# Five token blocks in place of six in a sliding-window attention and two-MLP kernel

## The reference

```
q, k, v: (4, 8, 576, 64)                   # batch, heads, sequence, head size
scores = q k^T / 8 - slope_h * |i - j|,    # only for 0 <= i - j < 128
attn   = softmax(scores) v                 # -> x: 2304 tokens x 512
h = relu(x @ w_in1); x = (h * h) @ w_out1  # 512 -> 2048 -> 512
h = x @ w_in2;       out = (h * cos(h)) @ w_out2
```

## Time and profile before

| | |
|---|---|
| median of 3 runs | 913.17 us (911.78 to 913.77) |
| the profiled execution | 912.75 us, its span 910.6 us |
| TensorE matmuls | 6128, busy 894.9 us |
| VectorE, ScalarE, GpSimd busy | 518.6, 369.2, 193.7 us |
| granted TensorE clock, mean | 0.998 of full |

### The profile page before, as it was taken

One profiled execution on the slowest core, in us unless ns is written; L12 is line 12 of the kernel. 1 busy time (PEld: TensorE's weight loads), 2 busy tenths in 40 slices (PEclk: granted clock), 3 DMA queues, 4 the chain that ended last, 5 costly groups with the idle time before them and its releaser, 6 DMA issues.

```text
span 910.6 us, 17307 instructions
## 1 busy us (share of the span) xinstructions
PE 894.9 (98%) x6128; PEld 840.7 (92%) x6128; DVE 518.6 (57%) x1239; ACT 369.2 (41%) x886; POOL 193.7 (21%) x298
## 2 busy tenths in 40 slices
PE   6999899999999999999999999999999999999998
PEld 4888799999999999999999989999999899999987
DVE  6888553333333332332353878777676776777675
ACT  7888232223232222222232344444444443443433
POOL 9888992000000000000069910000000000000000
PEclk9999999999999999999999999999999999999999
DMA  7776520000000000000134200100100100100101
GB/s 245 251 248 199 165 70 1 1 0 0 0 0 0 0 0 0 0 0 0 46 117 128 80 2 1 35 0 0 35 0 0 35 0 0 35 0 0 35 1 35
DMA packets 22922, 40.15 MB, mean 44 GB/s; under 512 B 3680, under 2 KB 8800, under 8 KB 22880
## 3 DMA queue, kind: packets, MB, share of 16 engines
q1 hardware_dynamic: 22016, 38.77, 13.1%
q10 hardware_dynamic: 864, 0.82, 0.3%
HBM read 34.87 MB, written 4.72 MB: 43 GB/s over the span
## 4 chain that ended last, share of the span: by engine, by line
PE 95%; DVE 2%; POOL 2%; issue 1%; ACT 0%; DVEq 0%; ACTq 0%; POOLq 0%
PE psum L497 43%; PE psum L531 22%; PE psum L516 21%; PE psum L458 4%; PE psum L416 3%; PE psum L370 2%; POOL probs L319 1%; PE psum L379 0%; DVE g_lo L773 0%; DVE work L811 0%; DVE pt L750 0%; POOL win_lo L325 0%; DVE work L804 0%; DVE work L814 0%; POOL bias L309 0%
## 5 line engine op out<-in xcount | busy, mean ns | idle before, releaser
L497 PE MATMUL psum<-xs,win_hi 128*128 (+1 forms) x1536 | 391.6, 335 | 0.0
L497 PEld LDWEIGHTS psum<-xs,win_hi 128*128 128x128 f32 x1536 | 279.4, 188 | 8.4
L497 PE MATMUL psum<-xs,win_lo 128*128 (+1 forms) x768 | 257.8, 336 | 0.0
L602 ACT ACTIVATE g_hi<-work 128x384 fp32r<-128x384 f32 x192 | 101.0, 526 | 218.6 <-DVE work L790 153.9
L773 DVE TENSOR_TENSOR g_lo<-work,g_hi 128x384 fp32r<-128x384 f32 x192 | 119.2, 621 | 57.4 <-ACT g_hi L602 57.4
L780 DVE SCALAR_TENSOR_TENSOR work<-psum,work 128x384 f32<-128x384 f32 x96 | 53.4, 557 | 170.6 <-ACT work L607 170.3
L497 PEld LDWEIGHTS psum<-xs,win_lo 128*128 128x128 f32 x768 | 144.1, 188 | 0.0
L531 PE MATMUL psum<-g_hi,wout_hi 128*128 128x384 f32 x384 | 128.3, 334 | 0.0
L531 PE MATMUL psum<-g_lo,wout_hi 128*128 128x384 f32 x384 | 128.3, 334 | 0.0
L531 PE MATMUL psum<-g_hi,wout_lo 128*128 128x384 f32 x384 | 128.3, 334 | 0.0
L607 ACT ACTIVATE work<-psum 128x384 f32<-128x384 f32 x96 | 47.1, 491 | 193.2 <-PE psum L497 193.2
(11 more groups left out here) (60 smaller groups left out, 955.5 us busy)
## 6 DMA issues: line engine op xcount, KB each, us to landing
win_raw<-w_in SPq DMA_DIRECT2D x32, 256.0 KB, 3.3
v_raw<-v SPq DMA_DIRECT2D x16, 512.0 KB, 3.2
wout_raw<-w_out SPq DMA_DIRECT2D x32, 256.0 KB, 3.3
q_raw<-q_t SPq DMA_DIRECT2D x15, 288.0 KB, 3.5
k_raw<-k_t SPq DMA_DIRECT2D x15, 288.0 KB, 4.7
out<-x SPq DMA_DIRECT2D x10, 192.0 KB, 1.9
out<-x SPq DMA_DIRECT2D x12, 128.0 KB, 1.7
out<-x SPq DMA_DIRECT2D x10, 64.0 KB, 1.6
```

The costliest lines, as they stand in the source:

```text
L497: last = pe.matmul(o, wi[:, f, w], xs[:, bass.ds(par, 1), part, k, :], start=(k == 0 and n == 0), stop=(k == DT - 1 and n == 2))
L602: act.activation(g_hi[:, f % HID_RING, :], work2[:, f % 2, :], ACT.Copy).then_inc(g_hi_ready, 1)
```

## The change

The blocks become five for each MLP, of 512, 512, 512, 384 and 384 tokens (`SIZES`, `STARTS`); `t` counts 0 to 9. Tiles are sized for 512 columns. `xs` holds only the high part of two blocks. The low part of x goes to `x_lo`, a second name for the memory of `x`, so the subtraction writes over the x that it reads. All loops over blocks are written out, with slices fixed when the kernel is built. In a block of 512 tokens ScalarE copies out the token groups 0 and 2 and VectorE 1 and 3, each as one piece of 512 columns. Waits count by `out_count` what was `t * 4` and the like.

```diff
-N = 384
-BLOCKS = TOKENS // N
+SIZES = [512, 512, 512, 384, 384]
+STARTS = [sum(SIZES[:i]) for i in range(len(SIZES))]
+BLOCKS = len(SIZES)
+N = max(SIZES)
...
+def pieces_of(size):
+    pieces = []
+    for c in range(size // P):
+        col = 0
+        while col < DM:
+            strip, off = divmod(c * DM + col, size)
+            w = min(DM - col, size - off)
+            pieces.append((c, col, strip, off, w))
+            col += w
+    return pieces
+
+DVE_CHUNKS = {512: (1, 3), 384: (1,)}
+ACT_PIECES = [[p for p in pieces_of(n) if p[0] not in DVE_CHUNKS[n]] for n in SIZES]
+DVE_PIECES = [[p for p in pieces_of(n) if p[0] in DVE_CHUNKS[n]] for n in SIZES]
...
+        x_at = [top[0]]
         x = place("x", [P, DT, TOKENS], F32)
+        x_lo = place("x_lo", [P, DT, TOKENS], F32R, x_at)
...
-        xs = place("xs", [P, 2, 2, DT, N], F32R)
-        rest_at = [top[0] - 2 * 4 * DT * N]
+        xs = place("xs", [P, 2, DT, N], F32R)
+        rest_at = [top[0] - 4 * DT * N]
...
+        def out_count(pieces, t):
+            if t <= BLOCKS:
+                return 1 + 2 * t
+            return 1 + 2 * BLOCKS + sum(len(p) for p in pieces[:t - BLOCKS])
...
-                    for n, (wi, part) in enumerate(((win_hi, 0), (win_hi, 1), (win_lo, 0))):
-                        last = pe.matmul(o, wi[:, f, w], xs[:, bass.ds(par, 1), part, k, :],
-                                         start=(k == 0 and n == 0), stop=(k == DT - 1 and n == 2))
+                    hi, lo = xs[:, t % 2, k, 0:size], x_lo[:, k, x_block(t)]
+                    for n, (wi, part) in enumerate(((win_hi, hi), (win_hi, lo), (win_lo, hi))):
+                        last = pe.matmul(o, wi[:, f, w], part, start=(k == 0 and n == 0), stop=(k == DT - 1 and n == 2))
...
-                            last = pe.matmul(psum[:, Y_BANK + d, 0:N], wo[:, f, w], g[:, r, :],
+                            last = pe.matmul(psum[:, Y_BANK + d, 0:size], wo[:, f, w], g[:, r, 0:size],
...
-            with pe.Fori(0, BLOCKS - 1) as t:
-                mlp_block(t, 0, 0)
-            mlp_block(BLOCKS - 1, 0, 1)
-            with pe.Fori(BLOCKS, 2 * BLOCKS - 1) as t:
-                mlp_block(t, 1, 1)
-            mlp_block(2 * BLOCKS - 1, 1, None)
+            for t in range(2 * BLOCKS):
+                mlp_block(t)
...
-                dve.tensor_tensor(xs[:, par, 1, d, :], x[:, d:d + 1, x_block(t, second)],
-                                  xs[:, par, 0, d, :].bitcast(F32), ALU.subtract).then_inc(xs_ready, 1)
+                dve.tensor_tensor(x_lo[:, d, x_block(t)], x[:, d, x_block(t)],
+                                  xs[:, t % 2, d, 0:SIZES[t % BLOCKS]].bitcast(F32), ALU.subtract).then_inc(xs_ready, 1)
...
+            for t in range(2 * BLOCKS):
+                for f in range(FT):
+                    mlp_step(t, f)
+                    if t > 0 and f == LATE - 1:
+                        (put_out if t > BLOCKS else put_y)(t - 1)
```

More of the change, by code:

```diff
@@ L218, in step, with x_block @@
             return t * FT + (f + more)
-        def x_block(t, second):
-            return bass.ds((t - BLOCKS if second else t) * N, N)
+        def x_block(t):
+            at, n = STARTS[t % BLOCKS], SIZES[t % BLOCKS]
+            return slice(at, at + n)
+        def out_count(pieces, t):
+            if t <= BLOCKS:
+                return 1 + 2 * t
+            return 1 + 2 * BLOCKS + sum(len(p) for p in pieces[:t - BLOCKS])
         def store(eng, t, made, pieces, i):
[L225 to L228, removed]
+            c, col, strip, off, w = pieces[t][i]
+            eng.wait_ge(made, out_count(pieces, BLOCKS + t) + i + 1)
+            eng.dma_start(out[STARTS[t] + c * P:STARTS[t] + c * P + P, col:col + w],
+                          x[:, strip, STARTS[t] + off:STARTS[t] + off + w]).then_inc(stored, 16)
         @block.sync
@@ L550, in _ @@
                     values(s - 3)
-                    hidden(0, s - PAIRS, 0)
+                    hidden(0, s - PAIRS)
                 if s == 2:
@@ L611, in relu_step, with cos_step @@
                     act.wait_ge(x_ready, PAIRS)
[L612 to L616, removed]
+                    if t + 1 == BLOCKS:
+                        act.wait_ge(out_dve, out_count(DVE_PIECES, 1))
+                    split_x(t + 1, SPLIT_AT.index(f))
+            def cos_step(t, f):
+                size = SIZES[t - BLOCKS]
                 if f > 0:
                     round_g(t, f - 1)
-                elif not (isinstance(t, int) and t == BLOCKS):
+                elif t > BLOCKS:
                     round_g(t - 1, FT - 1)
-                a = work1[:, f % 2, :]
+                a = work1[:, f % 2, 0:size]
                 act.wait_ge(angle_ready, (t - BLOCKS) * FT + (f + 1))
@@ L626, in cos_step, with mlp_step @@
                 act.activation(a, a, ACT.Sin, bias=half_pi[:, 0:1], scale=-1.0).then_inc(act_ready, 1)
-                if f in SPLIT_AT and not no_next:
-                    act.wait_ge(out_dve, (t - BLOCKS) * 2 + (1 + 4))
-                    split_x(t + 1, SPLIT_AT.index(f), 1)
+                if f in SPLIT_AT and t + 1 < 2 * BLOCKS:
+                    act.wait_ge(out_dve, out_count(DVE_PIECES, t + 2 - BLOCKS))
+                    split_x(t + 1, SPLIT_AT.index(f))
+            def mlp_step(t, f):
+                (cos_step if t >= BLOCKS else relu_step)(t, f)
             def put_y(t):
@@ L663, in _ @@
             act.sem_inc(out_act, 1)
[L664 to L684, removed]
+            for t in range(2 * BLOCKS):
[3 more added lines that the diff above has]
+                        (put_out if t > BLOCKS else put_y)(t - 1)
             last = 2 * BLOCKS - 1
-            for f in range(LATE, FT):
-                cos_step(last, f, 1)
             round_g(last, FT - 1)
             put_out(last)
-            for i in range(len(ACT_PIECES)):
+            for i in range(len(ACT_PIECES[last - BLOCKS])):
                 store(act, last - BLOCKS, out_act, ACT_PIECES, i)
@@ L791, in cos_g, with cos_step @@
                                   ALU.mult).then_inc(g_done, 1)
-            def cos_step(t, f, no_next):
-                before = (t, f - 1) if f > 0 else None if isinstance(t, int) and t == BLOCKS else (t - 1, FT - 1)
-                h = psum[:, H_BANK + f % HID_RING, 0:N]
-                k, w = work1[:, f % 2, :], work2[:, f % 2, :]
+            def cos_step(t, f):
+                size = SIZES[t - BLOCKS]
+                before = (t, f - 1) if f > 0 else None if t == BLOCKS else (t - 1, FT - 1)
+                h = psum[:, H_BANK + f % HID_RING, 0:size]
+                k, w = work1[:, f % 2, 0:size], work2[:, f % 2, 0:size]
@@ L817, in cos_step, with mlp_step @@
                     lo_g(*before)
-                if f in SPLIT_AT and not no_next:
-                    dve.wait_ge(out_act, (t - BLOCKS) * 2 + (1 + 4))
-                    split_x(t + 1, SPLIT_AT.index(f), 1)
+                if f in SPLIT_AT and t + 1 < 2 * BLOCKS:
+                    dve.wait_ge(out_act, out_count(ACT_PIECES, t + 2 - BLOCKS))
+                    split_x(t + 1, SPLIT_AT.index(f))
+            def mlp_step(t, f):
+                (cos_step if t >= BLOCKS else relu_step)(t, f)
             def put_y(t):
```

136 lines of the change are left out of this document (57 added, 79 removed).

## The result

The changed kernel takes 901.09 us (median of 4 runs, 900.71 to 901.46) against 912.95 us for the one before (4 runs, 911.78 to 913.77). The ratio is 0.9871, with a 95% interval of 0.9854 to 0.9888: 1.3% faster. The profiled execution took 901.46 us against 912.75, its span 899.5 against 910.6. The forecast was 901.5.

A forecast was written before the change was run, and what follows sets the result against it. TensorE bounds the kernel: matmul count times distance between starts. Terms -7.7 - 3.7 + 0.5 - 0.5 = -11.4 us from 912.75 give 901.4, stated as 901.5; range 899.8 to 906.0 us.

The forecast's parts named there:

- The fixed 13.3 ns for each matmul: Both MLPs: each matmul costs 13.3 ns above its columns at 2.4 GHz; 576 fewer matmuls give -7.7 us.
- Mixed steps of 384 and 512 columns: Second MLP steps mixing both widths cost 0.067 us extra each; 55 fewer such steps give -3.7 us.
- The wait at the first split: In `split_first`, longer subtractions make TensorE wait before `hidden(0, 0)`'s fourth quarter: +0.5 us, bounds 0 and 1.5 us.
- The stall at the switch: TensorE's wait for VectorE's `g_lo` after the switch of MLPs disappears: -0.5 us; bounds 0.5 kept or grown to 3.
- Borders, DMAs, tail: Copies at block borders stay covered, output stores lie off the path, the tail is unchanged: no cost.
- Rival A: The part above 2.4 GHz belongs to columns; every 512-column matmul takes 232.0 ns, MLPs gain nothing, 913 us; chance 0.09.
- Rival C: Written-out code adds at most 63 instruction packets; TensorE pausing at each costs 19.5 us, giving 921 us; chance 0.04.
- Rival B: Waits at the start and at the switch of MLPs grow to their bounds, giving 906 us; chance 0.07.

## Why the prediction was right

- The fixed 13.3 ns for each matmul, read from 23 starts at the kernel's end: right. 226.7 ns in both MLPs, 120.0 at 256 columns, and the gain is gone with the sizes alone. The rule of the Trainium skill (TensorE: Matmul & The Clock Gate, "Back-to-back issue gap"), 2.5 ns for each matmul, which that section calls the gap of an isolated matmul, has the right form and for these matmuls the wrong size: an estimate by it makes the 576 matmuls worth near 1.4 us. No run here shows why these have 13.3.
- Mixed steps of 384 and 512 columns at 0.067 us: right, 3.0 us for 46 fewer where 3.1 was expected, and 1.02 for 1.1. It is no constant of every change of width: with 256 columns it is 0.02, and no run shows why.
- Both together: of the MLP stretch's -11.30 us the wait for `x_lo` is +0.43 and the vanished stall -0.53, which leaves -11.20 for these two terms. The forecast had -11.4. The whole sum had -11.4 too, and -11.3 came.
- The wait at the first split: there, 0.43 us for 0.5, but at the second quarter where the step put it at the fourth. The four subtractions ended at 96.81, as forecast (96.8), but the second of them alone took 1.76 us (93.70 to 95.46 in VectorE's timeline), and the step hadn't looked at single ones. So the right size is partly luck. They grew from 3.48 to 4.26 us, by 1.22, not by 4/3; an undisturbed one grew from 0.56 to 0.69 us, by 1.23.
- The stall at the switch: gone as forecast, and GpSimd its cause, but by an easier road. The step "the slow step is at most 4/3 of 4.53, some 5.8 to 6.0 us" was a bound and it measured 4.86, once 5.28. What GpSimd adds to a step is 1.28 us (4.86 - 3.58), once 1.70, where it was 1.68 (4.53 - 2.85). VectorE doesn't fall back at all, where the forecast had 0.4 to 0.6 us a step.
- Borders, DMAs, tail: no wait, 4.3 us behind the last matmul in both kernels.
- Rival A (no gain) needed 232 ns in all matmuls of 512 columns; only the first nine behind a change show it. Rival C: 25 packets of instructions more, not 63, and no gap on TensorE in the stretches. Rival B's larger waits didn't come.
- The bounds of the range: the high one adds 3.5 us for the stall, but from a term of -0.5 to a stall that has grown to 3 us (2.5 more than before) it is 3.0, which gives 905.4 and not 906.0; the low one takes off 1.1 us for a scatter of 1.4. Neither was near the result. That the time came out within 0.4 us of 901.5 is closer than the scatter allows one to claim: the start of the first `hidden` alone moves by 1.8 us.

## What to carry to other kernels

Where one engine is full, divide a stretch by the count of its instructions at two sizes before believing in any rate. The distance of starts at two widths (384 and 512 columns here) splits a matmul into columns and a fixed part, and says what larger blocks are worth. Take the second size from a quiet, long run of equal instructions as well as from the mixture: their difference was a cost of its own, and reordering removed half of it without changing any work. Measure that cost for the widths at hand: 0.067 us for 384 and 512 columns was 0.02 for 256 and 512. When a block grows beside an engine that slows its neighbour, scale the neighbour's own work, not the slow-down: here, at two sizes, the part added by GpSimd didn't grow with the block.

## What the runs showed of the hardware

- Matmuls of 128 x 128 float32r weights, each with a weight load of 188 ns, start 120.0, 173.3 and 226.7 ns apart for 256, 384 and 512 columns: 13.3 ns over 2.4 GHz each time.
- After a change from 384 to 512 columns the distance swings for nine matmuls, after one back to 384 for six; the two cost 0.067 us together. A change from 256 to 512 and back costs 0.02.
- At 256 columns matmuls start 120.0 ns apart although each has a weight load of 192 ns.
- VectorE's step of six operations takes 2.85 us alone and 4.53 beside GpSimd's weight splitting at 384 columns, 3.58 and 4.86 (once 5.28) at 512. GpSimd's four operations take 4.52 and 4.87 us then.
- The same attention code reaches the first `hidden` between 92.6 and 94.4 us in ten profiled executions.
